# A fused linear-attention and two-layer feed-forward kernel on one core: layer 1 in 256-token sets, and every engine's program without loops

## The reference, cut to what matters

```python
for t in range(S):                                  # attention, per batch and head
    y[t]  = r[t] @ (state + outer(u * k[t], v[t]))
    state = w[t][:, None] * state + outer(k[t], v[t])
x = y.reshape(3072, 384)
x = (sigmoid(x @ w_gate) * (x @ w_val)) @ w_out      # layer 1, inner size 1536
h = x @ w_in                                         # layer 2, inner size 2048
out = where(h > 0, h, exp(min(h, 0)) - 1) @ w_out2
```

## Time and profile before

| | us |
|---|---|
| median of 3 runs | 1202.69 (1201.72 to 1202.88) |
| span of the profiled execution | 1203.3 |
| attention alone, up to the first layer-1 matmul | 0 to 94.1 |
| first mixed round (with 30 weight splits) | 94.1 to 230.0 |
| four more mixed rounds | 230.0 to 717.3 |
| layer 1 of the last block, alone | 717.3 to 793.8 |
| layer 2 | 793.8 to 1203.3 |

### The profile page before, as it was taken

One profiled execution on the slowest core, in us unless ns is written; L12 is line 12 of the kernel. 1 busy time (PEld: TensorE's weight loads), 2 busy tenths in 40 slices (PEclk: granted clock), 3 DMA queues, 4 the chain that ended last, 5 costly groups with the idle time before them and its releaser, 6 DMA issues.

```text
span 1203.3 us, 18133 instructions
## 1 busy us (share of the span) xinstructions
PE 1155.1 (96%) x6336; PEld 1006.2 (84%) x6336; DVE 669.5 (56%) x1044; ACT 472.2 (39%) x889; POOL 295.5 (25%) x290
## 2 busy tenths in 40 slices
PE   5778998999999999999999999999999999999999
PEld 4666777888888888888888888889999899899998
DVE  8777868494839393939393933354433334343433
ACT  2433444333333333333333333365544545454543
POOL 5563434143615351535153520000000000000000
PEclk9879998999999999999999999999999999999999
DMA  5451624122312231133204004220100101010000
GB/s 85 80 95 44 106 65 86 40 37 30 54 40 27 38 48 43 20 45 39 53 12 54 0 19 138 66 71 23 52 0 12 40 0 52 0 52 0 26 0 26
DMA packets 153413, 51.80 MB, mean 43 GB/s; under 512 B 126624, under 2 KB 148768, under 8 KB 153376
## 3 DMA queue, kind: packets, MB, share of 16 engines
q1 hardware_dynamic: 153376, 51.33, 21.0%
HBM read 41.88 MB, written 9.44 MB: 43 GB/s over the span
## 4 chain that ended last, share of the span: by engine, by line
PE 82%; DVE 11%; issue 4%; ACT 2%; DMA 0%; POOL 0%; DVEq 0%; SPq 0%; POOLq 0%; ACTq 0%
PE ps L606 21%; PE ps L639 17%; PE ps L631 16%; PE ps L615 10%; PE ps L544 7%; DVE RKW L828 6%; PE ps L560 3%; PE ps L534 3%; PE ps L565 2%; PE ps L573 2%; DVE hl L897 1%; DVE A L853 1%; DVE WS L917 1%; ACT RKW L669 1%; PE ps L581 1%
## 5 line engine op out<-in xcount | busy, mean ns | idle before, releaser
L606 PE MATMUL ps<-xh,WS 128*128 128x512 f32 x864 | 251.3, 408 | 1.6 <-DVE xl L888 1.6
L669 ACT ACTIVATE hh<-work 128x512 fp32r<-128x512 f32 x168 | 106.4, 633 | 287.5 <-DVE work L907 205.5
L544 PEld LDWEIGHTS ps<-RKW 128*128 128x128 f32 x1152 | 157.2, 203 | 59.1 <-DVE RKW L828 38.8
L544 PE MATMUL ps<-RKW 128*128 128x128 f32 x1152 | 167.6, 293 | 34.2 <-DVE RKW L828 34.0
L639 PE MATMUL ps<-WS,hh 128*128 128x384 f32 x768 | 198.0, 339 | 0.5 <-DVE hl L897 0.5
L828 DVE TENSOR_TENSOR RKW<-RKW,WL 64x256 f32<-64x256 f32 x288 | 186.1, 646 | 16.1 <-PE ps L544 13.7
L606 PEld LDWEIGHTS ps<-xh,WS 128*128 128x128 f32 x864 | 155.1, 190 | 30.7 <-issue 1.8
L897 DVE TENSOR_TENSOR hl<-work,hh 128x512 fp32r<-128x512 f32 x168 | 133.0, 791 | 85.3 <-ACT hh L669 84.3
L631 PE MATMUL ps<-xh,WS 128*128 128x512 f32 x576 | 164.2, 397 | 0.0
L615 PE MATMUL ps<-hh,WS 128*128 128x512 f32 x432 | 161.6, 411 | 0.4 <-DVE hl L897 0.3
L934 DVE SCALAR_TENSOR_TENSOR work<-work,ps 128x512 f32<-128x512 f32 x96 | 66.0, 688 | 172.2 <-ACT work L757 172.2
(11 more groups left out here) (67 smaller groups left out, 1324.7 us busy)
## 6 DMA issues: line engine op xcount, KB each, us to landing
nat<-in_w_dram SPq DMA_DIRECT2D x24, 192.0 KB, 3.7
nat<-in_k_dram SPq DMA_DIRECT2D x24, 192.0 KB, 4.8
nat<-in_r_dram SPq DMA_DIRECT2D x24, 192.0 KB, 5.2
V<-in_v_dram SPq DMA_DIRECT2D x24, 192.0 KB, 4.5
x_scratch<-work SPq DMA_DIRECT2D x6, 768.0 KB, 3.5
nat<-x_scratch SPq DMA_DIRECT2D x6, 768.0 KB, 5.2
out_dram<-Yt SPq DMA_DIRECT2D x5, 768.0 KB, 3.9
RKW<-in_moe_w_in_dram SPq DMA_DIRECT2D x16, 192.0 KB, 2.4
```

Of the source, the lines that this page charges most:

```text
L544: last = mm(bank[b][:, p * P:(p + 1) * P].rearrange("p (e i l) -> p e i l", e=2, l=L), K[:, g, :], Rb[:, :, :, 1, :], start=True, stop=True)
L606: last = mm(ps[:, VAL if val else GATE, :], gate_w(a, val, j, c), xp[b][:, c, :], start=(i == 0 and c == 0), stop=(i == 2 and c == KC - 1))
L669: return nc.scalar.activation(o, i, ACT.Copy)
```

## The change

Layer 1 works in sets of 256 tokens, one for each attention half, so 12 sets in place of 6. Matmuls of groups g, v and o have 256 columns; ACT's and DVE's instructions of layer 1 work on 256 columns; there are twice as many of each. Only half 0 of the attention comes ahead of set 0; set m (0 to 10) is mixed with the 24 parts of half m+1, and its transposes `transpose_x` (6 instead of 12) now stand inside the spread, behind third 96 of 102, rather than behind all thirds. Set 11 is alone. The part numbered s stands behind third 4s. The six early splits lie in L5, L6 and KT of half 0, and the other 30 behind the groups of set 0. Eight raw weight pieces have a place from the start (two in `sig` and `h`, two in the idle half of `Yt`), and the rest use the ring of four; the first sigmoid waits until the pieces in `sig` and `h` are split. x2 is stored half by half. SP loads half q within set q-2. All loops are written out, on every engine, layer 2's too; its arithmetic is as before.

```diff
-    ORDER = [(hf, name, i) for hf in range(HALF) for name in STAGES for i in range(2)] + \
-            [(0, "XT", i) for i in range(KC)]
+    HALVED = NB
+    TH = U * P
+    SETS = [(n, (hf,)) for n in range(HALVED) for hf in range(HALF)] + [(n, (0, 1)) for n in range(HALVED, NB)]
+    NS = len(SETS)
+    def cols(m):
+        return slice(SETS[m][1][0] * TH, (SETS[m][1][-1] + 1) * TH)
+    PARTS = [[("a", q, name, b) for name in STAGES for b in range(U)] for q in range(NQ)]
+    STREAM = [step for q in range(NQ) for step in PARTS[q] + ([ENDS[q]] if q in ENDS else [])]
...
+    PROGRAM = STREAM[:STREAM.index(("x", 0)) + 1]
+    for m in range(NS):
+        beside = STREAM[done:STREAM.index(("x", m + 1)) + 1 + MORE.get(m, 0)] if m + 1 < NS else []
...
+            PROGRAM += spread(THIRDS[m], beside, len(THIRDS[m]) - 1) + LATE[m]
...
-    EARLY = [len(FIRST) // 2 + 10 + 2 * x for x in range(AHEAD)]
+    EARLY = [("a", 0, name, b) for name in ("L5", "L6", "KT") for b in range(U)]
...
+    SPLIT2 = {("d", NS - 1, "v", j + 1, 2): j for j in range(F1 - 2)}
...
             def load_w1(first, end):
...
-                    if x >= NR1:
-                        sp.wait_ge(d_wlo, x - NR1 + 1)
+                    if x >= NR1 + ONCE:
+                        sp.wait_ge(d_wlo, x - (NR1 + ONCE if x < 2 * NR1 + ONCE else NR1) + 1)
...
-            def layer1(n, kind, j, i):
+            def layer1(m, kind, j, i):
+                t = cols(m)
...
-                        last = mm(ps[:, VAL if val else GATE, :], gate_w(a, val, j, c), xp[b][:, c, :],
+                        last = mm(ps[:, VAL if val else GATE, t], gate_w(a, val, j, c), xp[b][:, c, t],
...
-                        last = mm(ps[:, ACC + i, :], down_w(a, j, i), hp[b][:, j % 2, :],
+                        last = mm(ps[:, ACC + i, t], down_w(a, j, i), hp[b][:, j % 2, t],
...
-            with pe.Fori(1, NB - 1) as i:
-                mixed(i)
-            for step in LAST:
-                layer1(NB - 1, *step)
-            with pe.Fori(0, NB) as i:
+            for step in PROGRAM:
+                if step[0] == "a":
+                    attention(*step[1:])
+                elif step[0] == "x":
+                    transpose_x(step[1])
+                else:
+                    layer1(*step[1:])
+            for n in range(NB):
                 for step in STEPS2:
-                    layer2(i, *step)
+                    layer2(n, *step)
...
-                    nc.scalar.activation(sig, ps[:, GATE, :], ACT.Sigmoid).then_inc(a_sig, 1)
+                    if m == 0 and j == 0:
+                        act.wait_ge(d_wlo, NR1 + 2)
+                    nc.scalar.activation(sig[:, t], ps[:, GATE, t], ACT.Sigmoid).then_inc(a_sig, 1)
...
-                    tt(h, sig, ps[:, VAL, :], ALU.mult).then_inc(d_h, 1)
+                    tt(h[:, t], sig[:, t], ps[:, VAL, t], ALU.mult).then_inc(d_h, 1)
...
             def split_w1(x):
                 dve.wait_ge(a_whi, x + 1)
-                tt(w1_piece(x, 1), raw_w1[:, x % NR1, :], f32(w1_piece(x, 0)), ALU.subtract).then_inc(d_wlo, 1)
+                tt(w1_piece(x, 1), w1_raw(x), f32(w1_piece(x, 0)), ALU.subtract).then_inc(d_wlo, 1)
```

More of the change, by code:

```diff
@@ L233, in _, with load_half @@
         def _(sp):
[L234 to L238, removed]
+            def load_half(q):
+                n, hf = q // HALF, q % HALF
+                wait(sp, d_shift, q)
                 for x, src in ((2, w), (1, k), (0, r)):
-                    if first:
+                    if q == 0:
                         sp.wait_ge(d_zero, 3 - x)
@@ L332, in _ @@
-            load_shift(v, 1, 0)
+            load_v(0)
+            load_shift(v, 0)
+            load_w1(0, NR1 + ONCE)
+            load_half(1)
+            load_v(1)
+            load_w1(NR1 + ONCE, 2 * NR1 + ONCE)
+            load_shift(k, 1)
+            load_shift(v, 1)
             def split_until(step):
-                return AHEAD + sum(x[0] != "a" and x[-1] == 2 for x in MIXED[:MIXED.index(step)])
-            at = [NR1 + AHEAD] + [NR1 + split_until(("a", hf, name, 1)) for hf, name in ((0, "L4"), (0, "Y"), (1, "L4"))] + [N1]
+                return sum(PROGRAM.index(x) < PROGRAM.index(step) for x in SPLIT1)
@@ L364, in _ @@
-            load_half(NB - 1, 1)
-            load_v(NB - 1, 1)
-            load_shift(k, NB - 1, 1)
-            load_shift(v, NB - 1, 1)
-            store_x2(NB - 2)
-            sp.wait_ge(p_sw, 2 * HALF * NB)
-            sp.wait_ge(s_att, ATT_BLK * NB)
+            for m in range(NS - 1):
+                for q in range(3, NQ):
+                    if phase["a", q - 1, "L4", 1] == m:
+                        load_half(q)
+                        load_v(q)
+                        load_shift(k, q)
+                        load_shift(v, q)
+                store_x2(m)
@@ L372, in _ @@
+            sp.wait_ge(p_sw, 2 * NQ)
+            sp.wait_ge(s_att, len(USES))
             load_x2(0)
@@ L374, in _ @@
                 load_w2(j)
-            store_x2(NB - 1)
-            sp.wait_ge(x2_stored, 16 * (NB + 1))
-            with sp.Fori(0, NB - 1) as i:
-                load_x2(i + 1)
-                store_out(i)
+            store_x2(NS - 1)
+            for n in range(NB - 1):
+                load_x2(n + 1)
+                store_out(n)
             for b in range(B):
@@ L705, in attention, with transpose_x, layer1 @@
                         last.then_inc(a_rp, 1)
-                elif name == "XT":
-                    for c in range(KC):
-                        act.wait_ge(s_att, ATT_BLK * n + nth(hf, name, c))
-                        copy(xh[:, c, :], ps[:, attn_bank(hf, name, c), :]).then_inc(a_xhi, 1)
-            def layer1(n, kind, j, third):
+            def transpose_x(m):
+                t = cols(m)
+                for c in range(KC):
+                    act.wait_ge(s_att, count("x", m, c))
+                    copy(xh[:, c, t], ps[:, bank_of("x", m, c), t]).then_inc(a_xhi, 1)
+            def layer1(m, kind, j, third):
+                t = cols(m)
                 if third < 2:
@@ L762, in layer2 @@
                 elif kind == "x":
-                    if more:
+                    if n + 1 < NB:
                         split_x(n + 1)
                 elif j == F2 - 1:
-                    act.wait_ge(out_stored, 16 * (n + 1))
+                    wait(act, out_stored, 16 * n)
                     for b in range(0, B, 2):
@@ L829, in next_level_r, with attention @@
                 last.then_inc(d_r, 1)
-            def attention(n, hf, name, b):
-                q = 2 * n + hf
-                bank = [ps[:, attn_bank(hf, name, i), :] for i in range(KC if name == "XT" else 2)]
+            def attention(q, name, b):
+                hf = q % HALF
+                bank = ps[:, bank_of("a", q, name, b), :]
                 pairs = slice(b * PR, (b + 1) * PR)
```

461 lines of the change are left out of this document (194 added, 267 removed).

## The result

| | before | after |
|---|---|---|
| median of the runs | 1202.79 (1201.72 to 1205.14, 4 runs) | 1242.43 (1241.20 to 1244.42, 4 runs) |
| span of the profiled execution | 1203.3 | 1240.3 |
| first matmul of layer 1 | 94.1 | 53.1 |
| first set or round with splits | 135.9 | 81.5 |
| the rest of the mixed work | 487.3 | 650.3 |

A forecast was written before the change was run, and what follows sets the result against it. PE was busy for 1155.1 of 1203.3 us, with DVE the bound in the first mixed round. Start, set 0, ten phases, set 11 and layer 2: 52.9 + 82 + 647 + 42.3 + 409.5 = 1233.7, median 1233, range 1200 to 1254.

The forecast's parts named there:

- The start: Attention ahead of set 0: first layer-1 matmul at 52.9 us instead of 94.1, with six splits adding 2.5 us.
- One matmul: Layer 1 on PE: 119 ns for 256 columns, so the doubled matmuls cost 7.4 us more in all.
- The rival in which load and matmul collide: Layer-1 matmuls of 256 columns take 125 ns instead of 119: +23 us, 1256 us; chance 0.08.
- Set 0: First mixed set, with 30 weight splits: bound by DVE, 82 us.
- DVE above 85%: Expected sign in set 0: DVE busy for more than 85% of some 82 us.
- A phase: Each of sets 1 to 10: 61.0 us plus waits of 3.1 and 0.6, 64.7 us; ten make 647.
- DVE's backlog: In L1 to L3 of each phase, DVE needs 16.95 us against PE's 13.9, so PE waits about 3.1.
- Set 11: Last layer-1 set, alone: 38.6 us of matmuls, 3.1 waiting for layer-2 weights, 0.6 at the end; 42.3 us.
- Layer 2: The stretch after set 11 stays at 409.5 us.
- the 0.6: Last step of the sum: the runs' median taken as 0.6 us below the profiled span.
- no wait in the phases: Rival for sets 1 to 10: PE's order gives DVE enough time, phases 61.1, set 0 at 74, total 1186; chance 0.15.
- The clock rival: Each phase's waits lower the granted clock, adding 4 us ten times: 1273 us; chance 0.05.

The follow-up runs named there:

- experiments 2 to 4: The changed kernel with attention parts given more room in L1 to L3 (1208.31 us), seven eighths of masked score copies left out (1205.15), or parts packed closer (1273.66).
- kernel 6: The changed kernel with the first four layer-2 weight pieces loaded ahead of the last x2 store in SP's queue; 1240.50 us, ratio 1.0310 to the kernel before.
- experiment 7: The changed kernel with both more room for attention parts in L1 to L3 and early layer-2 weight loads; 1205.93 us, ratio 1.0024 to the kernel before.
- kernel 12: The changed kernel with parts strewn by their DVE work, transposes of x behind all thirds, and four layer-2 pieces loaded early; 1214.79 us, ratio 1.0066.
- kernel 4: As kernel 2, but with the parts of L1 to L3 packed closer (widths 1.2 instead of 6.3); 1273.66 us, ratio 1.0578 to the kernel before.
- kernel 8: The changed kernel with only block 0 in sets of 256 tokens, later sets of 512; 1211.93 us, ratio 1.0063 to the kernel before.
- kernel 2: The changed kernel with attention parts strewn by their DVE work, more room in L1 to L3, less elsewhere; 1208.31 us, ratio 1.0033 to the kernel before.

## Why the prediction was nearly right

It named the direction, the place and the engine. By its own steps, against the profiled execution:

- **The start**: 52.9 predicted, 53.07 measured; the waits of the six splits were not read one by one.
- **One matmul**: 119 ns from the line through 512 and 384 columns; 18 of them take 2.13 us, 118 ns. The rival in which load and matmul collide is refuted. By the Trainium skill's figure for 256 columns ("TensorE: Matmul & The Clock Gate", section "Back-to-back issue gap"), 109.2 ns, which the page gives for a matmul by itself, each would be 9 ns shorter than these rows have it.
- **Set 0**: 82 predicted, 81.5 measured, and that close by luck, for two errors cancel. DVE's work was put at 62.6 us (40, and 22.6 of splits) and measured 57.7, mostly because a split took 0.61 us in the mean and not 0.75. Its waits for ACT at the splits were put at 11 us and measured 15.2. The rest of its idle time is 8.6, against 8.5. So the sign "DVE above 85%" did not come: it is at 71%. The set also took 77.0 to 88.0 us in the profiles of the experiments.
- **A phase**: 64.7 predicted, 64.95 to 65.1 measured. The waits came to 3.7 us as predicted (3.1 in the levels and 0.55 at the end against 3.1 and 0.58), the rest to 61.3 in place of 61.0. In ten phases that is 3 us, the first of the two errors. Of the places named, v5 did not wait; v4, o4 and L1.1 did.
- **DVE's backlog** was the reason given for the 3.1, and experiments 2 to 4 show it: with room or with less work the waits go, with less room they grow. The two sums that it was made of hold: 8.04 + 4.75 us of attention jobs in L1 to L3 against the 13.1 taken, and low 3 waiting 0.5 us for ACT.
- **Set 11**: 42.3 predicted, 45.7 measured; this is the term that was mis-sized. The load and the wait of 3.1 us were right in kind (3.5 measured; landing at +8.85 against +8.2). Two things were missing: the clock at 0.55 behind the wait, 1.5 us, and the wait of 0.8 for the low part of layer 2's first x. These and 0.4 of the load make 2.7 of the 3.4; most of the rest is matmul time, for PE is busy for 39.5 us in this set of kernel 6, at clock 1.00, and not for 38.6. Experiment 6 took 5.0 us off this set by loading earlier, which is the load's wait together with the clock's fall.
- **Layer 2**: 409.5 and 409.7.

The sum of what was measured is 53.1 + 81.5 + 650.3 + 45.7 + 409.7 = 1240.3, 6.6 above the 1233.7: 3 from the phases, 3.4 from set 11. The runs' median lies 2 us above that span, not 0.6 below it as the prediction took it to. In every run whose span is on record, the time is 1.7 to 2.0 us above the span; so the execution profiled before must itself have taken about 1205, and the 0.6 set it against shorter ones. So some 2.7 of the 9.4 us by which 1233 falls short come from this step and not from the kernel.

Of the rivals, "no wait in the phases" (1186) fell twice. As a forecast of this kernel it is wrong by 56 us. As a price of the change without its waits, which is experiment 7, it is wrong by 16 to 20 us, and the reason is worth naming: it took a phase at 61.1 (61.97 measured), set 0 at 74 (78.1) and set 11 at 39 (40.6). In set 0 PE still waits for DVE even where the parts stand well, and DVE for ACT at the splits (15.0 us in kernel 7); the phases keep a wait at the end. PE is idle for 48 us in all before, which bounds what the order alone can give; kernel 7 still has 42 (PE is busy for 1157.9 of its 1200.1). In kernel 7 layer 1 starts 42 us earlier than before, but that is not what the change can return. Halves of the stretches before, with nothing added, come to 48.5 + 67.9 + 10 x 60.9 + 38.1 + 409.7 = 1173, 30 us less than before. Kernel 7 pays of these 3.4 us in the start (51.9), 10 in set 0 (78.1), 10.5 in the ten phases (61.97) and 2.5 in set 11 (40.6). In the phases 0.5 us each is PE's idle time; PE is busy for 61.45 us of one, against 60.4 for half a round before. Some 3 us are left.

The clock rival (1273) did not come about in this kernel: its ten phases are at 1.00, with a wait of 1.5 us in each. The clock did fall in two of the ten phases of kernel 12, and for a part of a third, where the longest wait is 0.9 us, and in six of the ten of kernel 4, behind a wait of 2.5. These runs do not show what decides between them.

## What to carry to other kernels

When independent work is strewn evenly beside a dense stream, sum the in-order jobs of the second engine stretch by stretch, not over the round: the same DVE work cost 65 us a phase evenly strewn and 62 weighted. Halving a tile halves the cover of every chain that doesn't halve with it, so look for the chains whose queue also carries other jobs. And before paying for an earlier start, work out what it can return with nothing added: here 30 us, and not the 42 by which layer 1 starts earlier.

## What the runs showed of the hardware

**Weight loads of the full array hide behind 256 columns.** 18 matmuls of 256 columns, each with a load of 128 x 128, take 2.13 us. One such matmul with its load costs 118 ns, half of the 234 for 512 columns to 1 ns.

**The granted clock of the same stretch differs from profile to profile, and this costs several us.** Set 0 has the same order and nearly the same DVE work (57.7 to 58.5 us) in three profiles: it took 81.5 us at clock 0.96 (after), 85.9 at 0.90 (kernel 6) and 86.8 at 0.88 (kernel 8). PE waits often in it, 14.9 us in all in the changed kernel. The steady phases of the changed kernel stay within 0.2 us of each other at 1.00. The start shows the difference most sharply. The stretches ahead of set 0 in kernel 2, where layer 1 began at 60.4:

```profile
0.00:40.00 40.00, 23.21 (x113) 20.37 (x113) 35.36 (x50) 12.59 (x28) 21.88 (x32) 0.86 0.60 108
40.00:50.00 10.00, 9.87 (x45) 9.47 (x46) 7.71 (x10) 3.81 (x9) 6.46 (x5) 0.50 1.13 188
50.00:60.40 10.40, 9.33 (x44) 8.56 (x43) 3.24 (x8) 1.15 (x3) 0.00 (x0) 0.55 0.17 32
```

and in kernel 7, whose start is the same code, where it began at 51.9:

```profile
0.00:40.00 40.00, 22.28 (x118) 20.00 (x119) 35.80 (x51) 12.72 (x28) 22.12 (x32) 0.83 0.63 110
40.00:51.90 11.90, 9.78 (x83) 8.93 (x81) 11.20 (x17) 4.68 (x11) 6.11 (x5) 1.00 0.99 178
```

In the first PE is busy all the time from 40 to 50 and gets 45 matmuls done at the lower level (0.50, which is 1.2 GHz); in the second it gets 83 done in 11.9 us at the higher. The first start is 8.5 us longer. The runs of one kernel part in the same way: those of kernel 7 at 1202 have a clock of 0.993, those at 1210 one of 0.984 to 0.987. Only one execution of each kernel has a profile, so where in the longer runs the clock fell is not known. A difference of less than these 8 us between two kernels is not to be read from a few runs, and a profile's span may not stand for the median: that of kernel 2 is its longest run of ten.

**A fall of the clock can follow a short wait or none that differs.** In kernel 12 two like phases of ten ran at 0.90, 6.4 us longer each, with a wait of 0.9 us that the phases at 1.00 have too. In kernel 4 six of ten fell behind a wait of 2.5 us, in the changed kernel none of ten with one of 1.5, and in its set 11 the clock was 0.55 from 1.3 us behind the wait of 3.5. What starts a fall at one wait and not at the same wait two phases earlier stays open.
